# Weight sets split in two pieces at two places of a step, in an attention and two-layer feed-forward kernel with seven-product matrix multiplication

## The chip, the cores and the metric

The kernel runs on one core of a Trainium2 chip. The metric is the device time of one execution in microseconds (us). Three executions of the kernel before took 1682.86, 1685.94 and 1686.4 us; the median is 1685.94.

## The reference

```python
kv = einsum('bhsd,bhse->bhde', k, v)              # batch 8, heads 8, seq 576, head_dim 64
out = einsum('bhsd,bhde->bhse', q, kv)
out = out / sqrt(mean(out * out, -1) + 1e-6) * g_norm
x = out.transpose(0, 2, 1, 3).reshape(4608, 512)
gate = 1 / (1 + exp(-(x @ w_gate)))               # w_gate, w_val: 512 x 1536
y = (gate * (x @ w_val)) @ w_out                  # w_out: 1536 x 512
h = y @ w_in                                      # 512 x 2048
g = where(h >= 1, h, where(h <= -1, 0, (h + 1) ** 2 / 4))
result = g @ w_out2                               # 2048 x 512
```

All of it is float32.

## The kernel before, in words

Each large float32 product is made from three matmuls of rounded parts: an operand is split into a high part (a cast on ScalarE, ACT) and a low part (operand minus high part, on VectorE, DVE), and TensorE (PE) adds low x high, high x low and high x high (`product`). On top of that the four large products are done block by block with seven products of half size instead of eight (numbered 1 to 7, in the order 1, 5, 6, 2, 7, 4, 3), whose operands are sums and differences of quarters. ACT copies some results out of PSUM (`p1_kept`, `u2_kept`, `u3_kept`), DVE adds others (`c11`, `c12`, `c22`).

There are four stages. A: x times w_gate and w_val, 96 steps (16 half blocks of tokens by 6 sets of output columns), with the attention of the next batches between its products in the first seven blocks. B: the gated result times w_out, 8 blocks. C: y times w_in, 64 steps (8 blocks by 8 sets). D: the last product, 18 units.

The sums of weight quarters are made as 34 tasks, one for each *weight set* of seven chunks of 256 columns. GpSimd (POOL) loads a set's four quarters into one of two stage buffers, makes three more chunks out of them in four sums (L657 to L664, L668 to L675), and then loads the set after the next into the buffer that has come free, once `v_ready` says that the set before is done. `split_weights(task)` on ACT (L733) casts the seven chunks of the stage into the ring `v_hi`, in one instruction of 1792 columns (L749); `split_weights(task)` on DVE (L1105) subtracts them into the ring `v_lo`, again in one instruction (L1108, recorded at `low`, L1097), and counts `v_ready` up by one.

The order of each engine is written out by hand; every engine runs its list in order and waits at semaphores. In stage A, ACT's step k is (L892 to L963): copy of product 1 (`p1_kept`, L900), sigmoid of the first half (L903), root or first items of the next block, **the weight set** (L910 to L915), copy of product 6 (`u2_kept`, L924), more items, `square_heads` and `split_square` of attention (L938), sigmoid of the second half (L945, it waits for `c12`), inverse (L947), copy of product 7 (`u3_kept`, L951). DVE's step k is (L1315 to L1405): `c22` (L1321), items, product of the first half (`h0_ready`, L1342), items, **the weight set** (L1357 to L1362), `c12` (L1371), an item, `c11` (L1380), `split_square` (L1382), `split_inverse` (L1384), product of the second half (`h_ready`, L1389), items.

PE's step k in stage A is: (k, 1), (k, 5), (k-1, 4), (k, 6), (k-1, 3), (k, 2), (k, 7), each six matmuls, where (k, n) is product n of step k. (k, 7) waits for `u2_kept`; (k, 5) waits for `c12` of the step before; (k-1, 3) waits for `c22`; attention's products stand between them. In the first six steps of the blocks 0 and 8, (k, 1) waits also for `v_ready`, that is for its own weight set (L1690).

Sets are made at these places: set 0 and set 1 ahead of the loop or in step 0; sets 2 to 5 in the steps 1 to 4 of stage A (the set made in step k is wanted by (k+1, 1)); sets 6 to 11 in the steps 40, 43, 45, 46, 49 and 50 (`SECOND_SETS`, wanted from step 48 on); sets 12 to 25 in fourteen steps from 53 to 87 (`FOLDS`), which SyncE stores to DRAM (L443 to L449) for stages B and D; sets 26 to 29 in stage B; sets 30 to 33 in the steps 0, 1, 3 and 4 of stage C (`THIRD_SETS`, wanted from step 4 on). In stage C the set stands near the end of the step on both engines: on ACT after the copies for `c21` and `u2_kept` (L1043), on DVE after `c12`, the clamp and `c11` (L1512).

Of the kernel before, what the change touches and what calls it, by code (L numbers as in the profile page):

```python
# [27 lines left out]
SEVEN = 7  # L28
# [39 lines left out]
def chunk_pieces(task):  # L68
    if task < A2_TASK:
        return parts(SEVEN * task, SEVEN)  # L70
    if task < FOLD1_TASK:
        return parts(42 + SEVEN * (task - A2_TASK), SEVEN)
    if task < C_TASK:

        return parts(28 + SEVEN * (task % 2), SEVEN)
    return parts(14 + SEVEN * (task - C_TASK), SEVEN)


# [8 lines left out]
def program(nc, kv_in, q_in, qrest_in, g_in, w1_in, w2_in, out):  # L87
# [15 lines left out]
    with ctx:  # L103
# [189 lines left out]
        def heads_of(k):  # L293
# [3 lines left out]
            return (n, c) if 2 <= n < B and c < K else None  # L297

        def mean_of(k):
            return heads_of(k - 1) if k else None  # L300
# [64 lines left out]
        def _(sp):  # L365
# [77 lines left out]
            def store_fold_hi(task):  # L443
                sp.wait_ge(v_hi_done, task + 1)
                sp.dma_start(fold_place(task, 0), fold_chunks(v_hi, task)).then_inc(fold_stored[task % 2], 16)

            def store_fold_lo(task):
                sp.wait_ge(v_ready, task + 1)
                sp.dma_start(fold_place(task, 1), fold_chunks(v_lo, task)).then_inc(fold_stored[task % 2], 16)  # L449
# [114 lines left out]
            for b in range(C_BLOCKS):  # L564

                sp.wait_ge(ct_ready, SEVEN * (b + 1))
                if b < C_BLOCKS - 1:
                    load_block(b + 1)
                else:
                    load_quarter(0, 1)  # L570
                for s in range(C_SETS):

                    if b == C_BLOCKS - 3 and s == 0:
                        sp.wait_ge(v_ready, TASKS)
# [34 lines left out]
        def _(pool):  # L609
# [99 lines left out]
            for task in range(TASKS):  # L709
# [10 lines left out]
                if 0 < task < TASKS - 1:  # L720
                    pool.wait_ge(v_ready, task)
                if task == C_TASK:
# [9 lines left out]
        def _(act):  # L732
            def split_weights(task):  # L733
                act.wait_ge(stage_summed, 4 * (task + 1))
# [11 lines left out]
                elif C_TASK <= task:  # L746
                    act.wait_ge(p_done[ORDER[min(task - C_TASK - 1, 6)]], C0)
                for base, first, count in chunk_pieces(task):
                    done = nc.scalar.copy(v_hi[:, base:base + count, :], stage[:, task % 2, first:first + count, :])  # L749
# [129 lines left out]
            for c in range(1, K):  # L879
                square_heads(0, c)  # L880
            split_weights(0)
            scale_heads(0, 1)
# [5 lines left out]
            for i in range(4):  # L888
                split_item(0, i)
            split_weights(1)  # L890

            for k in range(A_STEPS + 1):  # L892
# [15 lines left out]
                if s == 0 and b < A_BLOCKS:  # L908
                    split_item(b, 4)
                if 1 <= k < 5:  # L910
                    split_weights(1 + k)
                if k in SECOND_SETS:
                    split_weights(A2_TASK + SECOND_SETS[k])
                if k in FOLDS:
                    split_weights(FOLD1_TASK + FOLDS[k])  # L915
                if k == A_STEPS - 1:
# [18 lines left out]
                if k == 1:  # L935
                    square_heads(1, 2)
                    scale_heads(1, 2)
                if heads_of(k):  # L938
                    square_heads(*heads_of(k))
# [27 lines left out]
            for b in range(B_BLOCKS):  # L967
                for i, number in enumerate(ORDER):
# [24 lines left out]
                    if b == B_BLOCKS - 2 and i in (2, 4):  # L993
                        split_weights(C_TASK + i // 2 - 1)
                    if b == B_BLOCKS - 1:
                        if 2 <= i < 4:
                            split_weights(C_TASK + i)
                        elif i == 4:
# [10 lines left out]
            for k in range(C_STEPS + 1):  # L1009
                b, s = divmod(k, C_SETS)  # L1010
                g = C0 + k
                if k < C_STEPS:
                    act.wait_ge(p_done[1], g + 1)
                    act.wait_ge(c11_ready, g)
                    if k == 0:
                        act.wait_ge(c12_ready, C0)
                        act.wait_ge(c22_ready, C0)
                    nc.scalar.copy(c_kept[:, 0, :], X[k % 2][:, 0:C]).then_inc(p1_kept, 1)  # L1018
                if 0 < b < C_BLOCKS and s == 0:
                    split_c_item(b, 4)  # L1020
# [22 lines left out]
                if k in THIRD_SETS:  # L1043
                    split_weights(C_TASK + THIRD_SETS[k])
                if k == 60:
# [49 lines left out]
        def _(dve):  # L1095
# [8 lines left out]

            def split_weights(task):  # L1105
                dve.wait_ge(v_hi_done, task + 1)
                for base, first, count in chunk_pieces(task):
                    done = low(v_lo[:, base:base + count, :], stage[:, task % 2, first:first + count, :],  # L1108
# [185 lines left out]
            copy_kv(0)  # L1294
            split_weights(0)
            invert(0)
# [18 lines left out]
            for k in range(A_STEPS + 1):  # L1315
# [41 lines left out]
                if 1 <= k < 5:  # L1357
                    split_weights(1 + k)
                if k in SECOND_SETS:
                    split_weights(A2_TASK + SECOND_SETS[k])  # L1360
                if k in FOLDS:
                    split_weights(FOLD1_TASK + FOLDS[k])  # L1362
                if k == A_STEPS - 1:
# [21 lines left out]
                if k:  # L1385
                    tile = gate[:, (k - 1) % 2, 1, :]
                    dve.wait_ge(sig1_ready, k)
                    dve.wait_ge(c22_ready, k)
                    nc.vector.tensor_tensor(tile, c22[:], tile, ALU.mult).then_inc(h_ready, 1)  # L1389
                if s == 3 and b + 1 < B:  # L1390
                    normalize(b + 1, 3)
                if k == 0:
                    split_weights(1)
                    sum_item(0, 5)
# [16 lines left out]
            for b in range(B_BLOCKS):  # L1411
                for i, number in enumerate(ORDER):
# [20 lines left out]
                    if b == B_BLOCKS - 2 and i in (2, 4):  # L1433
                        split_weights(C_TASK + i // 2 - 1)
                    if b == B_BLOCKS - 1:
                        if 2 <= i < 4:
                            split_weights(C_TASK + i)
                        elif i == 4:
# [19 lines left out]
            for k in range(C_STEPS + 1):  # L1458
# [28 lines left out]
                elif k == C_STEPS - 2:  # L1487
                    sum_d_item(0, 2)
                if k:
                    dve.wait_ge(p_done[3], g)  # L1490
# [21 lines left out]
                if k in THIRD_SETS:  # L1512
                    split_weights(C_TASK + THIRD_SETS[k])
                if k == C_STEPS - 1:
# [41 lines left out]
        def _(pe):  # L1556
# [125 lines left out]
            def a_product(k, number, dst, start):  # L1682
# [6 lines left out]
                if number == 1 and b in (0, B):  # L1689
                    pe.wait_ge(v_ready, (A_SETS if b else 0) + s + 1)  # L1690
                chunk = ((42 if b >= B else 0) + SEVEN * s) % CHUNKS + QUAD[number]
# [90 lines left out]
            def c_product(k, number, dst, start):  # L1782
# [6 lines left out]
                if number == 1 and b == 0:  # L1789
                    pe.wait_ge(v_ready, C_TASK + s + 1)  # L1790
                chunk = (14 + SEVEN * s) % CHUNKS + QUAD[number]
# [100 lines left out]
```

## Time and profile before

| | |
|---|---|
| the profiled execution's own time | 1682.83 us |
| its span, first to last instruction | 1681.0 us |
| median of three timed executions | 1685.94 us (1682.86 to 1686.4) |
| mean granted PE clock | 0.995 of full |
| busy: ACT, POOL | 886.0 us (53%), 204.1 us (12%) |
| instructions | 31808 |
| DMA | 278.91 MB, 166 GB/s in the mean |

A matmul's duration in the timeline is longer than the distance between two of them, since they are pipelined. What an engine waited for stands in square brackets behind a row, with the us for which it was idle; PEld is PE's weight load, which runs beside the matmuls. L1097, L1100 and L1103 are helpers (a subtraction for a low part, an addition, a difference), so there the tile names say which work it is.

### The profile page before, as it was taken

To read this page: it belongs to the slowest core of one execution; us is meant where nothing else is said; L and a number is where in the kernel's file an instruction comes from. 1 tells how busy PE (TensorE), PEld (TensorE's weight loads), DVE (VectorE), ACT (ScalarE), POOL (GpSimd) and SP (SyncE) were. 2 spreads that over 40 slices of the span, in tenths; PEclk is the share of its full clock that TensorE was granted. 3 is DMA by queue.
4 is the path that set the end of the run, shared out by engine and by line. 5 is a ranking of instruction groups with operands and counts; after the bars stand their busy time and mean duration, and the time that the engine had idled before them with its cause. 6 is when DMAs were issued, how large, how long until landed. Compare 5 with 4: busy or idle time off the path is not lost. (4 is left out here: it accounts for less than half of the span.)

```text
span 1681.0 us, 31808 instructions
## 1 busy us (share of the span) xinstructions
PE 1653.5 (98%) x12473; PEld 1623.5 (97%) x12475; DVE 1219.3 (73%) x1725; ACT 886.0 (53%) x1612; POOL 204.1 (12%) x266
## 2 busy tenths in 40 slices
PE   8999999999999999999999999999999999999999
PEld 6799999999999999999999999999999989999999
DVE  4677776778787675877778887777777677676664
ACT  4666666655555554444445555555555444444442
POOL 3510000015432320200002410000001200000000
PEclk9999999999999999999999999999999999999999
DMA  7544434333776778745443433333438944444450
GB/s 259 161 127 145 149 133 145 116 128 132 249 252 227 246 243 279 245 140 154 130 141 139 163 128 131 117 121 141 165 141 272 334 151 138 140 135 126 126 131 34
DMA packets 229317, 278.91 MB, mean 166 GB/s; under 512 B 33072, under 2 KB 172848, under 8 KB 229168
## 3 DMA queue, kind: packets, MB, share of 16 engines
q1 hardware_dynamic: 217104, 233.35, 42.1%
q0 software_dynamic: 12064, 43.52, 7.9%
q8 instruction: 99, 1.62, 0.4%
q14 instruction: 50, 0.41, 0.1%
HBM read 156.76 MB, written 120.06 MB: 165 GB/s over the span
## 5 line engine op out<-in xcount | busy, mean ns | idle before, releaser
L1560 PE MATMUL x<-t_hi,v_lo 128*128 128x288 f32 x1664 | 497.0, 299 | 4.9 <-ACT c_kept L1018 1.8
L1561 PE MATMUL x<-t_lo,v_hi 128*128 128x288 f32 x1664 | 491.9, 296 | 0.0
L1562 PE MATMUL x<-t_hi,v_hi 128*128 128x288 f32 x1664 | 490.4, 295 | 0.0
L1560 PEld LDWEIGHTS x<-t_hi,v_lo 128*128 128x128 f32 x1664 | 313.0, 188 | 9.6 <-issue 2.6
L1562 PEld LDWEIGHTS x<-t_hi,v_hi 128*128 128x128 f32 x1664 | 314.2, 189 | 0.0
L1561 PEld LDWEIGHTS x<-t_lo,v_hi 128*128 128x128 f32 x1664 | 313.6, 188 | 0.1
L1560 PE MATMUL y<-t_hi,v_lo 128*128 128x288 f32 x832 | 248.8, 299 | 5.0 <-DVE c L1100 1.7
L1561 PE MATMUL y<-t_lo,v_hi 128*128 128x288 f32 x832 | 245.9, 295 | 0.0
L1562 PE MATMUL y<-t_hi,v_hi 128*128 128x288 f32 x832 | 245.2, 295 | 0.0
L1560 PE MATMUL x<-v_hi,t_lo 128*128 128x256 f32 x576 | 164.2, 285 | 4.2 <-ACT o_tile L1089 4.2
L1560 PEld LDWEIGHTS y<-t_hi,v_lo 128*128 128x128 f32 x832 | 156.4, 188 | 9.5 <-DVE c_tile L1100 3.1
L1561 PE MATMUL x<-v_lo,t_hi 128*128 128x256 f32 x576 | 163.9, 285 | 0.0
L1562 PE MATMUL x<-v_hi,t_hi 128*128 128x256 f32 x576 | 163.9, 285 | 0.0
L1562 PEld LDWEIGHTS y<-t_hi,v_hi 128*128 128x128 f32 x832 | 156.9, 189 | 0.0
L1561 PEld LDWEIGHTS y<-t_lo,v_hi 128*128 128x128 f32 x832 | 156.6, 188 | 0.1
L1097 DVE TENSOR_TENSOR t_lo<-gq,t_hi 128x1024 fp32r<-128x1024 f32 x90 | 109.7, 1222 | 61.3 <-ACT t_hi L872 61.3
L1097 DVE TENSOR_TENSOR t_lo<-hq,t_hi 128x864 fp32r<-128x864 f32 x112 | 118.3, 1080 | 30.3 <-ACT t_hi L841 30.3
L841 ACT CAST t_hi<-hq 128x864 fp32r<-128x864 f32 x112 | 99.8, 917 | 50.6 <-DVE hq L1103 25.7
L1560 PEld LDWEIGHTS x<-v_hi,t_lo 128*128 128x128 f32 x576 | 111.6, 194 | 4.4 <-ACT o_tile L1089 4.4
L1561 PEld LDWEIGHTS x<-v_lo,t_hi 128*128 128x128 f32 x576 | 111.6, 194 | 0.0
L1562 PEld LDWEIGHTS x<-v_hi,t_hi 128*128 128x128 f32 x576 | 111.5, 194 | 0.0
L872 ACT CAST t_hi<-gq 128x1024 fp32r<-128x1024 f32 x90 | 94.5, 1050 | 31.5 <-PE y L1562 23.4
(185 smaller groups left out, 3518.8 us busy)
## 6 DMA issues: line engine op xcount, KB each, us to landing
g_scratch<-c_tile SPq DMA_DIRECT2D x128, 288.0 KB, 2.4
gq<-g_scratch SPq DMA_DIRECT2D x64, 512.0 KB, 6.1
h_scratch<-gate SPq DMA_DIRECT2D x192, 144.0 KB, 1.9
hq<-h_scratch SPq DMA_DIRECT2D x32, 864.0 KB, 5.2
stage<-w_in POOLq DMA_DIRECT2D x68, 256.0 KB, 3.8
kv_ring<-kv_in SPq DMA_DIRECT2D x30, 512.0 KB, 4.4
fold_hi<-v_hi SPq DMA_DIRECT2D x14, 896.0 KB, 5.0
fold_lo<-v_lo SPq DMA_DIRECT2D x14, 896.0 KB, 6.7
```

Of the source, the lines that this page charges most:

```text
L841: nc.scalar.copy(b_slot(e)[0], b_source(i, hh)).then_inc(bt_hi_done, 1)
L872: nc.scalar.copy(d_slot(e)[0], d_source(u, i)).then_inc(s_hi_done, 1)
L1097: return nc.vector.tensor_tensor(out, raw, hi.bitcast(f32), ALU.subtract)
L1560: nc.tensor.matmul(dst, s_lo, m_hi, start=start, stop=False, skip_group_check=True)
L1561: nc.tensor.matmul(dst, s_hi, m_lo, start=False, stop=False, skip_group_check=True)
L1562: return nc.tensor.matmul(dst, s_hi, m_hi, start=False, stop=stop, skip_group_check=True)
```

## The change

`set_pieces(task, piece)` cuts the chunks of a set at the fourth: piece 0 is four chunks (1024 columns), piece 1 three chunks (768 columns). `split_weights` on both engines takes a piece and handles it alone. `v_hi_done` and `v_ready` now count pieces, so all that wait for a set wait for twice the number; DVE's piece waits for ACT's same piece. In stage A piece 0 stands where the set stood, and piece 1 later in the step: on ACT after the items and attention's extra work of step 1, ahead of `square_heads`; on DVE after the product of the second half (L1389) and ahead of `normalize(b + 1, 3)` and the last items. In stage C piece 1 stands where the set stood, and piece 0 earlier: on ACT right after the copy of product 1 (L1018), on DVE ahead of `c12`. Sets 0, 1 and 26 to 29 are made in two pieces at their one place.

```diff
+def set_pieces(task, piece):
+    low, high = ((0, 4), (4, SEVEN))[piece]
+    cut = [(base, first, max(first, low), min(first + count, high)) for base, first, count in chunk_pieces(task)]
+    return [(base + start - first, start, end - start) for base, first, start, end in cut if end > start]
...
+        def weight_task(k):
+            if 1 <= k < 5:
+                return 1 + k
+            if k in SECOND_SETS:
+                return A2_TASK + SECOND_SETS[k]
+            return FOLD1_TASK + FOLDS[k] if k in FOLDS else None
...
             def store_fold_hi(task):
-                sp.wait_ge(v_hi_done, task + 1)
+                sp.wait_ge(v_hi_done, 2 * (task + 1))
             def store_fold_lo(task):
-                sp.wait_ge(v_ready, task + 1)
+                sp.wait_ge(v_ready, 2 * (task + 1))
...
                 if 0 < task < TASKS - 1:
-                    pool.wait_ge(v_ready, task)
+                    pool.wait_ge(v_ready, 2 * task)
...
-            def split_weights(task):
+            def split_weights(task, piece):
...
-                for base, first, count in chunk_pieces(task):
+                for base, first, count in set_pieces(task, piece):
                     done = nc.scalar.copy(v_hi[:, base:base + count, :], stage[:, task % 2, first:first + count, :])
                 done.then_inc(v_hi_done, 1)
...
# ACT, stage A: in place of the set
+                if weight_task(k) is not None:
+                    split_weights(weight_task(k), 0)
...
                 if k == 1:
                     square_heads(1, 2)
                     scale_heads(1, 2)
+                if weight_task(k) is not None:
+                    split_weights(weight_task(k), 1)
                 if heads_of(k):
                     square_heads(*heads_of(k))
...
# ACT, stage C
                     nc.scalar.copy(c_kept[:, 0, :], X[k % 2][:, 0:C]).then_inc(p1_kept, 1)
+                if k in THIRD_SETS:
+                    split_weights(C_TASK + THIRD_SETS[k], 0)
...
                 if k in THIRD_SETS:
-                    split_weights(C_TASK + THIRD_SETS[k])
+                    split_weights(C_TASK + THIRD_SETS[k], 1)
...
# DVE
-            def split_weights(task):
-                dve.wait_ge(v_hi_done, task + 1)
-                for base, first, count in chunk_pieces(task):
+            def split_weights(task, piece):
+                dve.wait_ge(v_hi_done, 2 * task + piece + 1)
+                for base, first, count in set_pieces(task, piece):
...
# DVE, stage A: piece 0 in place of the set, and
                     nc.vector.tensor_tensor(tile, c22[:], tile, ALU.mult).then_inc(h_ready, 1)
+                if weight_task(k) is not None:
+                    split_weights(weight_task(k), 1)
                 if s == 3 and b + 1 < B:
                     normalize(b + 1, 3)
...
# DVE, stage C
                 elif k == C_STEPS - 2:
                     sum_d_item(0, 2)
+                if k in THIRD_SETS:
+                    split_weights(C_TASK + THIRD_SETS[k], 0)
                 if k:
                     dve.wait_ge(p_done[3], g)
...
                 if k in THIRD_SETS:
-                    split_weights(C_TASK + THIRD_SETS[k])
+                    split_weights(C_TASK + THIRD_SETS[k], 1)
...
# PE, stages A and C
-                    pe.wait_ge(v_ready, (A_SETS if b else 0) + s + 1)
+                    pe.wait_ge(v_ready, 2 * ((A_SETS if b else 0) + s + 1))
-                    pe.wait_ge(v_ready, C_TASK + s + 1)
+                    pe.wait_ge(v_ready, 2 * (C_TASK + s + 1))
```

## Rows read from the trace of the kernel before

**Rows 1.** The page, busy time of the engines: us, share of the span, instructions.

```profile
PE 1653.5 (98%) x12473; PEld 1623.5 (97%) x12475; DVE 1219.3 (73%) x1725; ACT 886.0 (53%) x1612; POOL 204.1 (12%) x266
```

**Rows 2.** Busy us (instructions) of PE, PEld, DVE, ACT, POOL in a window; PEclk; DMA; GB/s.

```profile
1000.00:1070.00 70.00, 70.00 (x527) 70.00 (x526) 52.23 (x79) 38.05 (x71) 0.00 (x0) 1.00 0.39 144
```

**Rows 3.** Waits of PE over the span: releaser, us in all, times, longest.

```profile
PE y L1560 <- DVE c L1100: 1.7, 2, 1.6
...
PE x L1560 <- DVE v_lo L1097: 1.3, 2, 0.7
...
PE y L1560 <- DVE gate L1100: 1.3, 2, 1.1
```

**Rows 4.** Groups by line and shape: count, busy us, mean ns, idle us before.

```profile
L1097 DVE TENSOR_TENSOR t_lo<-gq,t_hi 128x1024 fp32r<-128x1024 f32 x90 | 109.7, 1222 | 61.3 <-ACT t_hi L872 61.3
...
L872 ACT CAST t_hi<-gq 128x1024 fp32r<-128x1024 f32 x90 | 94.5, 1050 | 31.5 <-PE y L1562 23.4 <-DVE gq L1103 6.3 <-PE h L1562 1.8
...
L1097 DVE TENSOR_TENSOR v_lo<-stage,v_hi 128x1792 fp32r<-128x1792 f32 x34 | 70.3, 2068 | 14.7 <-ACT v_hi L749 14.7
...
L749 ACT CAST v_hi<-stage 128x1792 fp32r<-128x1792 f32 x34 | 57.3, 1686 | 2.0 <-POOL stage L664 1.9
...
L1100 DVE TENSOR_TENSOR gate<-y,kept 128x288 f32<-128x288 f32 x96 | 43.2, 450 | 53.3 <-PE y L1562 53.3
```

**Rows 5.** Timeline, end of step 2 of stage A: start us, us, instruction, idle before.

```profile
62.89 1.95 DVE L1097 TENSOR_TENSOR v_lo<-stage,v_hi 128x1792 fp32r<-128x1792 f32 x1
...
65.24 0.45 ACT L945 ACTIVATE gate<-gate 128x288 f32<-128x288 f32 x1 [1.25 <-DVE gate L1100]
...
65.43 0.29 PE L1560 MATMUL x<-t_hi,v_lo 128*128 128x288 f32 x1
...
66.52 0.46 DVE L1389 TENSOR_TENSOR gate<-c,gate 128x288 f32<-128x288 f32 x1
...
66.55 0.53 PE L1648 MATMUL h<-inv_pair,spread_r 48*128 48x288 f32 x2 [0.16 <-DVE inv_pair L1097]
```

**Rows 6.** Timeline, step 4 of stage A.

```profile
81.07 2.57 DVE L1097 TENSOR_TENSOR v_lo<-stage,v_hi 128x1792 fp32r<-128x1792 f32 x1
...
81.71 2.51 POOL L660 TENSOR_TENSOR stage<-stage 128x256 f32<-128x256 f32 x1
...
82.36 0.67 ACT L780 CAST ps_hi<-sq 128x576 fp32r<-128x576 f32 x1
...
83.78 0.37 PE L1560 MATMUL x<-t_hi,v_lo 128*128 128x288 f32 x1 [0.71 <-DVE v_lo L1097]
...
84.29 1.25 DVE L1097 TENSOR_TENSOR ps_lo<-sq,ps_hi 128x576 fp32r<-128x576 f32 x1
...
85.59 0.34 PE L1633 MATMUL m<-ps_lo,head_r 128*48 128x288 f32 x1 [0.78 <-DVE ps_lo L1097]
```

**Rows 7.** Timeline, steps 59 and 60 of stage A.

```profile
466.98 0.40 PE L1560 MATMUL y<-t_hi,v_lo 128*128 128x288 f32 x1 [1.09 <-DVE gate L1100]
...
467.81 0.75 DVE L1097 TENSOR_TENSOR t_lo<-t_sum,t_hi 128x576 fp32r<-128x576 f32 x1
...
468.70 0.37 PE L1560 MATMUL x<-t_hi,v_lo 128*128 128x288 f32 x1
```

**Rows 8.** Timeline, steps 1, 4 and 5 of stage C.

```profile
952.22 0.37 PE L1560 MATMUL y<-t_hi,v_lo 128*128 128x288 f32 x1 [1.52 <-DVE t_lo L1097]
...
970.96 0.30 PE L1560 MATMUL x<-t_hi,v_lo 128*128 128x288 f32 x1
...
971.28 1.69 ACT L749 CAST v_hi<-stage 128x1792 fp32r<-128x1792 f32 x1 [1.61 <-POOL stage L664]
...
975.39 0.40 PE L1560 MATMUL x<-t_hi,v_lo 128*128 128x288 f32 x1 [0.56 <-ACT c_kept L1018]
```

**Rows 9.** Windows behind two long waits, columns as in rows 2.

```profile
668.00:675.00 7.00, 4.81 (x23) 4.45 (x23) 5.74 (x10) 3.09 (x6) 1.51 (x3) 0.76 0.36 110
...
947.00:953.00 6.00, 3.24 (x23) 2.80 (x22) 3.42 (x4) 2.69 (x4) 1.09 (x2) 1.00 0.07 15
```

More of the change, by code:

```diff
@@ L573, in _ @@
                     if b == C_BLOCKS - 3 and s == 0:
-                        sp.wait_ge(v_ready, TASKS)
+                        sp.wait_ge(v_ready, 2 * TASKS)
                         all_stored(sp, g_stored, C_SETS * b, 32)
@@ L880, in _ @@
                 square_heads(0, c)
-            split_weights(0)
+            split_weights(0, 0)
+            split_weights(0, 1)
             scale_heads(0, 1)
@@ L889, in _ @@
                 split_item(0, i)
-            split_weights(1)
+            split_weights(1, 0)
+            split_weights(1, 1)
             for k in range(A_STEPS + 1):
@@ L909, in _ @@
                     split_item(b, 4)
[L910 to L915, printed above, removed]
+                if weight_task(k) is not None:
+                    split_weights(weight_task(k), 0)
                 if k == A_STEPS - 1:
@@ L993, in _ @@
                     if b == B_BLOCKS - 2 and i in (2, 4):
-                        split_weights(C_TASK + i // 2 - 1)
+                        for piece in range(2):
+                            split_weights(C_TASK + i // 2 - 1, piece)
                     if b == B_BLOCKS - 1:
                         if 2 <= i < 4:
-                            split_weights(C_TASK + i)
+                            for piece in range(2):
+                                split_weights(C_TASK + i, piece)
                         elif i == 4:
@@ L1294, in _ @@
             copy_kv(0)
-            split_weights(0)
+            split_weights(0, 0)
+            split_weights(0, 1)
             invert(0)
@@ L1356, in _ @@
                         sum_item(b + 1, 5)
[L1357 to L1362, printed above, removed]
+                if weight_task(k) is not None:
+                    split_weights(weight_task(k), 0)
                 if k == A_STEPS - 1:
@@ L1389, in _ @@
                     nc.vector.tensor_tensor(tile, c22[:], tile, ALU.mult).then_inc(h_ready, 1)
+                if weight_task(k) is not None:
+                    split_weights(weight_task(k), 1)
                 if s == 3 and b + 1 < B:
@@ L1392, in _ @@
                 if k == 0:
-                    split_weights(1)
+                    split_weights(1, 0)
+                    split_weights(1, 1)
                     sum_item(0, 5)
@@ L1433, in _ @@
                     if b == B_BLOCKS - 2 and i in (2, 4):
-                        split_weights(C_TASK + i // 2 - 1)
+                        for piece in range(2):
+                            split_weights(C_TASK + i // 2 - 1, piece)
                     if b == B_BLOCKS - 1:
                         if 2 <= i < 4:
-                            split_weights(C_TASK + i)
+                            for piece in range(2):
+                                split_weights(C_TASK + i, piece)
                         elif i == 4:
```

## The prediction

> **What bounds the kernel now.** Read the page's first part first: TensorE (PE) is busy for 98% of the span [rows 1], so of 1681.0 us it stands still for 27.5. The other engines matter only where PE waits for them. Where it does not wait, a matmul costs 70.00/527 = 0.133 us [rows 2] and a product of six 0.80. Next, the waits of PE, a short list: for a weight set's low part, which is what this change moves, twice, 1.3 us together; for a gate half, 1.3 us; for `c22` twice, 1.7 us, of which 1.6 is one wait near the end of stage A [rows 3]. What a better place for the pieces could win is in such lines. Last, the order of time around the steps that hold a weight set: what PE is given next, and how early it was ready. I call product n of step k (k, n).
>
> **The operations.** A whole set is 1792 columns, one cast of 1686 ns on ScalarE and one subtraction on VectorE, 2068 ns in the mean. The first piece is 1024 columns; the trace has this shape as a cast of 1050 ns and a subtraction of 1222 ns; an addition such as `c12` takes 450 ns [rows 4]. The 768 columns between the two shapes cost 0.83 ns each on ScalarE and 1.10 on VectorE; so the second piece, 256 columns fewer than the first, is 1050-212 = 840 ns and 1222-282 = 940 ns. The sums are 1.89 against 1.69 us and 2.16 against 2.07: 34 sets make +6.8 and +3.1 us of busy time. Neither engine sets the end (53% and 73% of the span [rows 1]), so this costs only where one of them is late. No set wraps round the ring of 56 chunks (all bases are multiples of 7), so each piece is one instruction. The doubled counts ask for the whole set as before: PE, SyncE's stores and GpSimd's next load all wait for the second piece.
>
> What counts is the place. In VectorE's order the first piece stays ahead of the additions that PE waits for (`c12`, `c11`), which can come 0.8 us earlier; the second piece moves behind them and behind the product of the second half (L1389), which waits for ScalarE's second sigmoid. GpSimd gets the stage buffer 1 to 3 us later, and has the room: a set is loaded two sets ahead.
>
> **Step 2 of stage A.** The set made here is wanted by the first product of step 3. Before, the subtraction starts at 62.89 and ends at 64.84, and (3,1) starts at 65.43 without a wait [rows 5]. After: first piece until 64.1, `c12` until 64.5, `c11` until 64.9; the sigmoid starts at 64.6 instead of 65.24; from its start to that of L1389 there were 1.28 us (the inverse's cast and subtraction lie between), so L1389 starts at 65.9 and ends at 66.3, the second piece at 67.2. (3,1) starts at 67.3, 1.9 later. Behind it PE waited 0.3 us for the inverse (65.43+0.80 = 66.23, started 66.55), which is then ready: net **+1.6**. It is at least 1.2, if additions and inverse gain 0.4 more than I gave them, and at most 2.2, if L1389 gets no earlier at all: 66.52+0.46+0.94 = 67.9.
>
> **Step 4.** Here PE already waits 0.71 us for the low part and starts (5,1) at 83.78; then it waits 0.78 for the low part of the squares, until 85.59 [rows 6]. After: first piece 81.07 to 82.3, both additions until 83.1. On ScalarE the second cast stands ahead of the squares; the first ends 0.64 earlier, the second adds 0.84, so their high part ends at 83.2 where it ended at 83.03. Their subtraction (0.75 if undisturbed) ends at 84.1, L1389 at 84.6, the second piece at 85.4 to 85.5. (5,1) starts there, 1.6 to 1.7 later, but the mean square can follow 0.80 behind it, at 86.2 instead of 85.59: **+0.6**. Bounds: +0.3, if these operations overlap more than their durations say; +1.3, if a GpSimd sum comes between.
>
> On that there is a row and a rule. GpSimd's 256-column sum at 81.71 took 2.51 us, and the subtraction beside it 2.57, where the mean is 2.07 [rows 4, 6]: they hold each other up. The Trainium skill, page "SBUF — State Buffer", section "SBUF: two separate sides", says that VectorE instructions with two SBUF inputs and GpSimd's share one port pair as an exclusive lock, kept for a whole instruction. By that rule, the trace agreeing with it, cutting the subtraction gives GpSimd a gap to get in, and the second piece could wait for one more sum; this step would be nearer its upper bound.
>
> **Steps 0, 1 and 3.** Step 0 makes its set in two pieces in one place, and PE waits for it: +0.1 (0 to 0.2). By the reckoning of step 2 the second piece ends in step 1 just when (2,1) can start (0 to +0.4), and in step 3 well before (4,1), which has attention's products ahead of it: 0 for both. For set 0 the root leads on, not the set: 0.
>
> **Later sets of stage A.** All are made at least three steps ahead of use, so the late second piece harms nothing directly. What could be won is a wait of PE behind a long subtraction. The largest, 1.09 us at 466.98 (step 59), is for `c12`, queued behind it [rows 7]. With the first piece alone `c12` comes 0.8 earlier and PE starts (60,5) at 466.2. But two products later (60,6) started at 468.70, right after VectorE's next item (467.81+0.75 = 468.56), and VectorE has the same work before that item, plus 0.1 us. So the wait only moves: 0, between -0.2 and +0.2; likewise in step 53. In step 46 the shorter of the two `c22` waits (1.7-1.6 = 0.1 [rows 3], and as much again for the restart) goes, since the set no longer pushes what follows: -0.3, at least 0.
>
> **The start of stage C.** Set 30's subtraction began after a wait for a store; `c22` and an item stood behind it, and PE waited 1.52 us until 952.22 [rows 8]. The first piece now lies in the time in which VectorE waits anyway, so (0,3) starts about 1.1 earlier (the second piece alone, 0.94, stands before `c22`, instead of 2.07), and GpSimd loads as much earlier. But set 33, in step 4 of this stage, waits 1.61 us for GpSimd's last sum, until 971.28; its cast stood behind the copies for `c21` and `u2_kept`, and now its first piece stands ahead of them. With the sum 1.1 earlier the piece ends at 971.2, the copies at 972.0, and (4,7), which started at 970.96, starts there. Then (5,1), (5,5), (4,4) follow without gaps, and (5,6) starts at 972.0+3.2 = 975.2 against 975.39, where the 0.56 before it goes. Of the 1.1, 0.2 is left, and GpSimd's sums may fall better: **-0.3**, bounds -1.1 (sum 0.9 earlier still) and +0.7 (sum hardly earlier).
>
> **Sum.** 1.6+0.6+0.1-0.3-0.3 = +1.7 us. The profiled execution took 1682.83 us (span 1681.0), so 1684.5 in its state; it lies at the lowest of the three timed runs, 3.1 below their median of 1685.94. On the median it is 1687.6. All lower bounds give -0.1, all upper ones +5.0. The sum is within 0.2% (3.4 us), about what a measurement of this kernel can tell from no change.
>
> **Rivals.**
> - *The clock falls.* Behind the wait of 1.6 us near 670 [rows 3] the granted clock averaged 0.76 over 7 us, so 1.7 us of full speed were lost in a stretch at 1.2 instead of 2.4 GHz; behind the 1.52 us at 952 it did not fall [rows 9]. The new wait in step 2, or that in step 4, can do the same: +1.7+1.7 = +3.4, with both +5.1. This is the case on the slower side, and it decides from one fall on. The Trainium skill, page "TensorE: Matmul & The Clock Gate", section on the clock gate, calls the low level the default, which activity releases; both rows are open to that, and it names no other price here. The 3.1 us between timed runs may be such falls.
> - *Slower by the waits alone.* Steps 2 and 4 and stage C at their upper bounds, 2.2+1.3+0.7, and nothing won in step 46: +4.3. For it: GpSimd's held-up sum [rows 6, 8]. Against: three bounds at once.
> - *Faster.* The waits at 467 and 952 go and nothing comes behind them (-0.8, -1.5), that of 0.56 at 975 too, with -0.3 of step 46, and steps 0, 2 and 4 cost their lower bounds, +1.5: -1.7; with one clock fall of the span missing (1.7), -3.4, just where it would be told as faster. Against: the item behind 467 [rows 7], the sum at 971 [rows 8].
> - *Nothing:* the second pieces of steps 2 and 4 are hidden after all, 0. Against: (3,1) started 0.6 us after the low part, and the second piece moves behind three operations [rows 5].
>
> **Chances.** Forecast (+1.7, from -0.1 to +3.3) 0.60; clock fall 0.17, of it 0.09 beyond 3.4; slower by the waits alone 0.08; faster 0.07, of it 0.04 at 3.4 or beyond; nothing 0.08. So faster 0.04, slower 0.17, same 0.79. Range 1683.5 to 1690.8: from 1 below the forecast in the profiled execution's state to the median with the higher clock case nearly in full.
>
> **What would show it.** Right: a wait of PE for `v_lo` of some 1.5 to 2 us near 65 to 67 and another near 84; the wait at 467 short, with one for `t_lo` two products on; the wait at 952 below 0.6 us, and one near 970 for the copy of L1033; 68 casts and 68 subtractions of about 1.05/0.84 and 1.22/0.94. Wrong: (3,1) without a wait; no wait at 970; the wait at 467 gone with none behind it.

## The result and the profile after

The changed kernel took 1690.49 us (median of 11 runs, 1684.48 to 1692.97), the kernel before 1683.63 us (median of 11, 1678.05 to 1689.45). The ratio is 1.0033, 95% interval 1.0020 to 1.0046: slower by 0.33%, some 5.6 us. The forecast was +1.7 us and "within 0.2%"; the time lies inside the range given (1683.5 to 1690.8), 0.3 us below its upper end.

The profile is of an execution of 1684.48 us, the shortest of the eleven. Its mean granted clock was 0.997; in the others it was 0.991 (1692.97 us) to 0.996, which is 1.4 us for each 0.001; a line through all runs, each kernel about its own mean, has the same slope. The two profiled executions differ by 1.65 us where the medians differ by 6.9. In the trace before the granted clock was at its lower level for 3.4 us from 29.5, 36.3 and 671.2 us and for 6.8 us from 1350.4; in the trace after for 3.4 us from 44.5, 88.9 and 1355.3. So the trace after is one with few such falls: it shows the places where time went, not how often the clock falls.

The page, busy time of the engines:

```profile
PE 1651.2 (98%) x12473; PEld 1621.3 (96%) x12475; DVE 1221.7 (73%) x1759; ACT 891.5 (53%) x1646; POOL 203.4 (12%) x266
```

Waits of PE over the span (releaser, us in all, times, longest). The two waits for `v_lo` of 1.3 us together [rows 3] have become three of 6.4:

```profile
PE x L1584 <- DVE v_lo L1117: 6.4, 3, 3.5
...
PE x L1584 <- DVE t_lo L1117: 2.2, 3, 1.6
PE m L1604 <- DMA kv_ring<-kv_in: 2.2, 1, 2.2
...
PE y L1584 <- DVE c L1120: 1.9, 2, 1.6
...
PE x L1584 <- ACT c_kept L1053: 1.2, 1, 1.2
```

Groups by shape (count, busy us, mean ns, idle us before). The casts add 6.6 us to ScalarE (35.5+28.4-57.3), as forecast. The subtractions add 11.0 to VectorE (42.3+39.0-70.3), where 3.1 were forecast: the second piece takes 1146 ns in the mean, not 940 (worked out from [rows 4]). Of the 34 second pieces 21 took 0.95 us and one 1.13; twelve took 1.47 to 1.49, and each of these began 0.15 to 0.3 us after a sum of GpSimd had begun. VectorE's busy time as a whole rose by 2.4 us only, since other instructions were held up less (L1389, now L1406: 48.5 us before, 45.5 after, for 96):

```profile
L1117 DVE TENSOR_TENSOR v_lo<-stage,v_hi 128x1024 fp32r<-128x1024 f32 x34 | 42.3, 1243 | 8.4 <-ACT v_hi L765 8.4
L1117 DVE TENSOR_TENSOR v_lo<-stage,v_hi 128x768 fp32r<-128x768 f32 x34 | 39.0, 1146 | 0.0
...
L765 ACT CAST v_hi<-stage 128x1024 fp32r<-128x1024 f32 x34 | 35.5, 1044 | 2.3 <-POOL stage L679 2.3
...
L765 ACT CAST v_hi<-stage 128x768 fp32r<-128x768 f32 x34 | 28.4, 836 | 0.0
```

**Step 2 of stage A.** VectorE and, last, PE on the timeline (start us, us, instruction, idle before). This answers to [rows 5]: both additions, the inverse, the second product (L1406), and only then the second piece, for which (3,1) waits:

```profile
63.64 1.15 DVE L1117 TENSOR_TENSOR v_lo<-stage,v_hi 128x1024 fp32r<-128x1024 f32 x1
64.71 0.44 DVE L1120 TENSOR_TENSOR gate<-y,kept 128x288 f32<-128x288 f32 x1
...
65.98 0.52 DVE L1117 TENSOR_TENSOR inv_pair<-inv,inv_pair 16x288 fp32r<-16x288 f32 x1 [0.47 <-ACT inv_pair L821]
66.54 0.46 DVE L1406 TENSOR_TENSOR gate<-c,gate 128x288 f32<-128x288 f32 x1
66.91 0.95 DVE L1117 TENSOR_TENSOR v_lo<-stage,v_hi 128x768 fp32r<-128x768 f32 x1
...
68.01 0.37 PE L1584 MATMUL x<-t_hi,v_lo 128*128 128x288 f32 x1 [1.68 <-DVE v_lo L1117]
```

**Step 4.** The same, with GpSimd's sums beside it; it answers to [rows 6]. Three VectorE operations that overlap a sum are long (1.01, 0.97, 1.47 us), and (5,1) waits 3.55 us. The last row is of the trace before, where L1389 was as long beside a sum:

```profile
83.49 1.22 DVE L1117 TENSOR_TENSOR v_lo<-stage,v_hi 128x1024 fp32r<-128x1024 f32 x1
...
85.59 1.01 DVE L1117 TENSOR_TENSOR ps_lo<-sq,ps_hi 128x576 fp32r<-128x576 f32 x1 [0.15 <-ACT ps_hi L796]
86.53 0.97 DVE L1406 TENSOR_TENSOR gate<-c,gate 128x288 f32<-128x288 f32 x1
87.43 1.47 DVE L1117 TENSOR_TENSOR v_lo<-stage,v_hi 128x768 fp32r<-128x768 f32 x1
...
85.46 0.99 DVE L1389 TENSOR_TENSOR gate<-c,gate 128x288 f32<-128x288 f32 x1
```

```profile
85.95 1.24 POOL L677 TENSOR_TENSOR stage<-stage 128x256 f32<-128x256 f32 x1
87.27 0.82 POOL L679 TENSOR_TENSOR stage<-stage 128x256 f32<-128x256 f32 x1
```

```profile
89.05 0.58 PE L1584 MATMUL x<-t_hi,v_lo 128*128 128x288 f32 x1 [3.55 <-DVE v_lo L1117]
89.42 0.44 PE L1585 MATMUL x<-t_lo,v_hi 128*128 128x288 f32 x1
```

The matmul at 89.42 takes 0.44 us where others take 0.29: the clock has fallen, from 88.9 on, just before the wait ended. The window around it (columns as in [rows 2]) has a mean granted clock of 0.57; over 9 us around the end of step 2's wait it stayed whole:

```profile
66.00:75.00 9.00, 7.32 (x48) 6.12 (x47) 5.91 (x12) 3.25 (x7) 3.41 (x6) 1.00 0.54 178
...
88.50:92.50 4.00, 3.45 (x15) 3.31 (x16) 2.77 (x5) 0.74 (x2) 1.09 (x2) 0.57 0.78 214
```

What step 4 cost in all shows between two products of attention that lie ahead of it and behind it. In the trace before (the first two rows) they start at 79.72 and 103.76, 24.04 us apart; here (the other two) 26.04 apart, so **+2.0**:

```profile
79.72 0.29 PE L1560 MATMUL h<-pq_hi,kv_lo 128*128 128x288 f32 x1
...
103.76 0.29 PE L1560 MATMUL h<-pq_hi,kv_lo 128*128 128x288 f32 x1
...
82.14 0.29 PE L1584 MATMUL h<-pq_hi,kv_lo 128*128 128x288 f32 x1
...
108.18 0.29 PE L1584 MATMUL h<-pq_hi,kv_lo 128*128 128x288 f32 x1
```

**Stage C.** The products that answer to [rows 8], and the cast of set 33. The first row is of the trace before:

```profile
949.64 0.40 PE L1560 MATMUL x<-t_hi,v_lo 128*128 128x288 f32 x1 [1.24 <-ACT c_kept L1018]
...
953.07 0.40 PE L1584 MATMUL x<-t_hi,v_lo 128*128 128x288 f32 x1
...
954.57 0.37 PE L1584 MATMUL y<-t_hi,v_lo 128*128 128x288 f32 x1 [0.44 <-DVE t_lo L1117]
...
974.36 0.40 PE L1584 MATMUL x<-t_hi,v_lo 128*128 128x288 f32 x1 [1.17 <-ACT c_kept L1053]
...
977.90 0.40 PE L1584 MATMUL x<-t_hi,v_lo 128*128 128x288 f32 x1
```

```profile
972.66 1.05 ACT L765 CAST v_hi<-stage 128x1024 fp32r<-128x1024 f32 x1 [2.28 <-POOL stage L679]
```

From the product ahead of (0,3) to (5,6) it is 977.90-953.07 = 24.83 us; before, that product started at 949.64, so 975.39-949.64 = 25.75. Stage C gained 0.9 there, and 0.3 more in two short stops of PE before the products behind that are gone: **-1.2**. The wait for a copy near 974 is there, as forecast. The 1.24 us that PE waited just ahead of the product at 949.64 are gone too, but the change has no part in that: of the fourteen traces of this case six have this wait (1.1 to 1.7 us), e4 below among them, which is the change but for two guards, and eight don't, e11 among them, whose stage C is that of before.

**A wait that nobody expected.** In the trace after, VectorE waited 2.26 us near 647 for a store of a gate tile to land, and the products behind it came 1.0 us later:

```profile
647.20 0.46 DVE L1120 TENSOR_TENSOR gate<-z,kept 128x288 f32<-128x288 f32 x1 [2.26 <-DMA h_scratch<-gate]
```

It costs 0.8 to 1.4 us in six of the fourteen traces (the change, e3, e4, e5, e7, e9) and is in none of the others. e5 has all sets of stage A whole, so the late pieces don't make it; what these six share is the set of step 4 of stage C in two places, 300 us later. Why the store lands late stays open.

### The profile page after: what moved, and what is told of

It is laid out like the page before. It is cut to its first block and busy times, and to the rows that moved or that the text cites. A ratio compares the mean times of both kernels' runs of the same rounds, so it can differ in the third digit from the quotient of the medians.

```text
span 1682.7 us, 31904 instructions
## 1 busy us (share of the span) xinstructions
PE 1651.2 (98%) x12473; PEld 1621.3 (96%) x12475; DVE 1221.7 (73%) x1759; ACT 891.5 (53%) x1646; POOL 203.4 (12%) x266
```

## The experiments

Each kernel is the change with up to four settings: APART_A, the steps of stage A whose set has its second piece at the late place (in the others the pieces stand one behind the other at the early place, on ScalarE and VectorE); APART_C, the same for steps 0, 1, 3, 4 of stage C; WHOLE, the sets that stay one instruction and count for two; and the guards of GpSimd's sums of sets 1 and 2 (`pool.wait_ge(v_ready, 1)` and `2`). The change had left these two counts as they were, so set 2's sums began when half as much was done: at 32.91 us in the trace after, at 42.10 in that of before. A run's ratio is to the kernel before on the same chip. The medians of before were 1683.17, 1687.56 and 1684.28 us for the first, second and third group of four.

| kernel | median us | ratio, 95% | wait for `v_lo`, step 2 | step 4 | start of a clock fall at step 4's wait |
|---|---|---|---|---|---|
| the change | 1690.49 | 1.0033 (1.0020..1.0046) | 1.68 | 3.55 | 88.9 us |
| e1_together | 1686.09 | 1.0020 (1.0009..1.0031) | none | 1.32 | none |
| e2_early | 1689.21 | 1.0028 (1.0015..1.0041) | 1.68 | 3.55 | 89.1 |
| e3_no_early | 1683.04 | 0.9999 (0.9988..1.0010) | none | 1.31 | none |
| e4_guard | 1689.11 | 1.0030 (1.0017..1.0043) | 1.61 | 3.55 | 89.9 |
| e5_c_only | 1685.17 | 0.9992 (0.9978..1.0006) | none | 0.70 | none |
| e6_whole01 | 1684.07 | 0.9991 (0.9979..1.0002) | none | 1.31 | none |
| e7_pool | 1691.04 | 1.0037 (1.0021..1.0052) | 1.67 | 2.23 | 87.0 |
| e8_step4 | 1686.70 | 1.0005 (0.9990..1.0020) | none | 3.58 | 87.5 (6.8 us long) |
| e9_after_c11 | 1685.40 | 1.0005 (0.9992..1.0018) | 0.20 | 1.46 | none |
| e10_best | 1682.30 | 0.9985 (0.9972..0.9998) | none | 0.70 | none |
| e11_step2 | 1683.70 | 1.0002 (0.9986..1.0018) | 1.61 | 0.70 | none |
| e12_together2 | 1686.48 | 1.0010 (0.9996..1.0024) | none | 1.31 | none |

**First group: which of the places costs.**

```
e1_together:  APART_A = ()                 APART_C = ()            guards 2 and 4
```

> Every set in two pieces, but both pieces at the one place where the whole set stood, and GpSimd's two guards ahead of sets 1 and 2 doubled like all other counts. So only the instruction count differs from the kernel before. Theory A (the late second pieces of steps 2 and 4 of stage A cost the time): within 1 us of the kernel before, ratio 0.9995 to 1.0008. Theory B (68 more instructions and the cuts themselves cost): most of the measured 5.6 us, ratio about 1.003. Theory C (GpSimd's guards, which the change left at 1 and 2): as A, 1.000.

```
e2_early:     APART_A = (1, 2, 3, 4)       APART_C = ()            guards 2 and 4
```

> As the kernel with both pieces together, but in the steps 1 to 4 of stage A the second piece stands late, as in the change. Theory A: this alone brings the whole loss, ratio 1.002 to 1.0045; its trace has a wait of the tensor engine for v_lo of 1.5 to 2 us near 66 and one of 2.5 to 3.7 near 85. Theory B: ratio as of both pieces together, plus nothing. Theory C: 1.000 to 1.001.

```
e3_no_early:  APART_A = all but 1 to 4     APART_C = (0, 1, 3, 4)  guards as in the change
```

> The change, but in the steps 1 to 4 of stage A both pieces stand together in the old place. Theory A: the loss is gone and the gain of stage C is left, ratio 0.998 to 1.000; no wait for v_lo above 1 us near 66 and 85. Theory B: still 1.003. Theory C (guards, as in the change): still about 1.003.

```
e4_guard: the change, and in GpSimd's loop
-                    pool.wait_ge(v_ready, 1)
+                    pool.wait_ge(v_ready, 2)
...
-                    pool.wait_ge(v_ready, 2)
+                    pool.wait_ge(v_ready, 4)
```

> The change, but GpSimd's two guards wait for 2 and 4 pieces, that is for the whole sets 0 and 1 as before. Theory A: as the change, ratio 1.002 to 1.0045, with the waits for v_lo near 66 and 85. Theory C (the sums of set 2, which ran at 33 to 37 us instead of 42 to 46 and slowed three subtractions from 0.75 to 1.28 us, cost the time): 1.000 to 1.001.

Without the late pieces of steps 1 to 4 the whole loss is gone (e3, 0.9999, its interval clear of that of the change and of e4); with them and no other late piece it is nearly all there (e2, 1.0028). The guards are worth nothing that shows (e4 as the change). e1, with no piece at a late place, is still 0.2% slower, so the medians of e1 and e2 alone would leave little for the late pieces. Its trace is 3.5 us longer than that of before, and 2.6 of that arise in the first 62 us, where it waits 3.6 us for `kv_ring` against 0.8. These first 62 us differ from those of before by -1.2 (e3) to +7.3 us (e9) among the traces, whatever the pieces do. e1 was run again below.

**Second group: stage C, the first sets, and what is in step 4.**

```
e5_c_only:    APART_A = ()    APART_C = (0, 1, 3, 4)   WHOLE = sets 0 to 29           guards 2 and 4
```

> Only stage C's sets 30 to 33 in two pieces at two places; all others whole as in the kernel before. Theory A (early sets cost, stage C gains, the rest is neutral): ratio 0.998 to 1.000, and stage C's first six steps 1 to 2.5 us shorter; set 33's first piece waits for GpSimd and the tensor engine waits 1.2 us for the copy of product 6 near 970. My prediction had -0.3 us for stage C. Theory D (cutting set 0 lets GpSimd load set 2 earlier, against attention's kv loads): does not apply here, no kv wait above 1 us near 34.

```
e6_whole01:   APART_A = ()    APART_C = ()             WHOLE = sets 0 and 1           guards 2 and 4
```

> Both pieces together in one place everywhere, but sets 0 and 1 whole as before. The kernel with all pieces together measured 1.0020, with a wait of 3.6 us for kv_ring near 36. Theory D (the cut of set 0 ends it 0.5 us earlier, GpSimd's load of set 2 starts earlier and kv_ring's loads land later): ratio 0.9995 to 1.0005 here, kv wait back to 0.8 us. Theory B (more instructions cost): 1.002 as with all together. Theory E (the kv wait varies from run to run whatever the sets do): 1.002, with any kv wait.

```
e7_pool: the change, and GpSimd's sums of set 6 wait until set 5 is done
                 elif task == 2:
                     pool.wait_ge(v_ready, 2)
+                elif task == A2_TASK:
+                    pool.wait_ge(v_ready, 2 * A2_TASK)
```

> The change, but GpSimd makes the sums of set 6 only after set 5 is wholly done, so none of its sums runs beside step 4's second piece. Theory A1 (the order of VectorE's list costs, GpSimd's sums lengthen it by 1 us, and a fall of the clock follows the wait of 3.7 us): the wait for v_lo near 85 goes from 3.7 to 2.3 to 2.9 us; the fall of the clock near 89 stays or goes; ratio 1.001 to 1.003. Theory A2 (GpSimd is no part of it): wait 3.7 and ratio as the change, 1.003.

```
e8_step4:     APART_A = (4,)  APART_C = ()             WHOLE = all sets but set 5     guards 2 and 4
```

> All sets whole as in the kernel before but set 5, whose second piece stands late in step 4. Theory A: the wait for v_lo near 83 to 87 is 3 to 3.7 us with a fall of the clock behind it, +2 us or ratio 1.001 to 1.002. If the wait of step 2 is needed for the size of that of step 4: wait about 2.5, ratio 1.000 to 1.001.

e7 separates what made step 4's wait so long. Its VectorE and PE rows, with no sum beside them:

```profile
85.06 0.76 DVE L1132 TENSOR_TENSOR ps_lo<-sq,ps_hi 128x576 fp32r<-128x576 f32 x1
85.73 0.45 DVE L1425 TENSOR_TENSOR gate<-c,gate 128x288 f32<-128x288 f32 x1
86.10 0.95 DVE L1132 TENSOR_TENSOR v_lo<-stage,v_hi 128x768 fp32r<-128x768 f32 x1
```

```profile
87.20 0.58 PE L1605 MATMUL x<-t_hi,v_lo 128*128 128x288 f32 x1 [2.23 <-DVE v_lo L1132]
```

0.76, 0.45 and 0.95 us against 1.01, 0.97 and 1.47 of the changed kernel, 1.29 us together; the wait is shorter by 1.32. So the sums made 1.3 us of it. But the time didn't come back (its ratio, 1.0037, is even above the 1.001 to 1.003 expected): the clock fell all the same,

```profile
86.80:90.20 3.40, 3.00 (x12) 2.86 (x13) 3.33 (x5) 0.95 (x3) 3.00 (x3) 0.53 0.56 178
```

and a wait of 1.28 us for `pq_lo` near 101 us came in. The two attention products are 26.33 us apart (81.61, 107.94), no less than in the changed kernel. The sums had only moved: they now ran beside the subtraction for `pq_lo`, which took 1.27 us instead of 0.75. What such a hold-up costs the kernel, other traces show: in the five where `pq_lo` was held up without a late piece in step 4 (e3, e5, e6, e11, e12; waits of 1.28 to 1.30 us) the two products are 24.33 to 24.46 us apart, in the four where it was not (before, e1, e9, e10; 0.58) 23.98 to 24.05. So it costs 0.3 to 0.4 us. e8 has the fall with set 5's late piece alone:

```profile
88.97 0.58 PE L1603 MATMUL x<-t_hi,v_lo 128*128 128x288 f32 x1 [3.58 <-DVE v_lo L1130]
```

```profile
87.20:94.00 6.80, 5.03 (x21) 4.88 (x22) 4.00 (x6) 1.19 (x3) 2.51 (x5) 0.52 0.47 157
```

its distance is 26.99 us. Its ratio (1.0005) can't be told from that of no change, so for step 4 alone the trace is the evidence, not the median.

e5 (0.9992) came out as expected, with the waits of stage C as in the change. e6 (0.9991) came out just below the 0.9995 to 1.0005 expected, but not for the reason given: its wait for `kv_ring` was 1.8 us, not back to 0.8.

**Third group: order or place, the best version, and the repeat.**

```
e9_after_c11: the change, and in VectorE's loop of stage A
+                if 1 <= k < 5:
+                    split_weights(weight_task(k), 1)
                 if heads_of(k):
                     split_square(*heads_of(k))
...
-                if weight_task(k) is not None:
+                if weight_task(k) is not None and k >= 5:
                     split_weights(weight_task(k), 1)
```

> The change, but in steps 1 to 4 of the run-in VectorE makes the second piece of the subtraction right after the item's combining addition (c11), ahead of the split of the squares (split_square), split_inverse and the second product. Theory 'order' (the loss of steps 2 and 4 comes from where the second piece stands behind VectorE's other work of the item): the wait for v_lo near 66 us falls from 1.68 to 0.3 to 0.8 us, that near 85 us from 3.55 to 1.2 to 1.6 us, there is no stretch at half the clock near 89 us, and the ratio to before is 0.9985 to 1.001. Rival (the two places cost by themselves, by contention or by the cast, wherever VectorE's piece stands): a wait of over 2.5 us near 85 to 89 us and the clock fall stay, and the ratio is 1.003 as that of the change.

```
e10_best:     APART_A = ()    APART_C = (0, 1, 3)      WHOLE = sets 0 to 29 and 33    guards 2 and 4
```

> All sets whole at their old place as before, but sets 30, 31 and 32 of the start of stage C made at two places, and set 33 whole at its old place (GpSimd's guards doubled, so its sums run where they did before). Theory (the change's only gain is the start of stage C, about 1.2 us from step C0 to C8, and set 33's own late first piece costs part of it): that stretch at 45.0 to 46.2 us against 47.36 before, no wait for v_lo near 970 us, and a ratio of 0.998 to 0.9995. Rival (what stage C gains is lost again in a later wait): 1.000.

```
e11_step2:    APART_A = (2,)  APART_C = ()             WHOLE = all sets but set 3     guards 2 and 4
```

> All sets whole as before, but set 3 alone with its second piece late in step 2 of the run-in. Theory (step 2 costs by itself what the changed profile shows, a wait for v_lo of 1.68 us at 68 us, and no clock fall follows a wait of this length): a wait of 1.6 to 1.7 us near 66 to 68 us, the stretch from step 2 to step 4 about 1.1 us longer than 18.8 us, no clock fall between 66 and 75 us, and a ratio of 1.0003 to 1.001. Rival (the wait only takes the place of others): the stretch the same within 0.3 us and a ratio of 1.000.

```
e12_together2: as e1_together
```

> The same kernel as e1_together, run again: every set's cast and subtraction cut into four and three chunks, the two pieces one right after the other at the old place. It came out at 1.0020 [1.0009, 1.0031] the first time. If cutting itself costs that, it is 1.0015 to 1.0025 again; if that was the spread of the start of the kernel (waits for the first transfers and the clock falls of the first 50 us), it is 0.999 to 1.001.

In e9 the second piece stands right behind the addition for `c11`, and PE's two waits shrink to 0.20 (less than the 0.3 to 0.8 expected) and 1.46 us:

```profile
73.06 0.37 PE L1605 MATMUL x<-t_hi,v_lo 128*128 128x288 f32 x1 [0.20 <-DVE v_lo L1130]
```

```profile
90.40 1.45 DVE L1130 TENSOR_TENSOR v_lo<-stage,v_hi 128x768 fp32r<-128x768 f32 x1
91.78 1.28 DVE L1130 TENSOR_TENSOR ps_lo<-sq,ps_hi 128x576 fp32r<-128x576 f32 x1
```

```profile
92.00 0.37 PE L1605 MATMUL x<-t_hi,v_lo 128*128 128x288 f32 x1 [1.46 <-DVE v_lo L1130]
```

```profile
88.00:96.00 8.00, 6.45 (x48) 5.99 (x47) 8.00 (x11) 5.30 (x12) 5.63 (x6) 1.00 0.69 241
```

The clock stayed whole and the attention products are 23.98 us apart (87.19, 111.17), as before the change. The second piece is as long as ever here (1.45 us, a sum beside it), and ScalarE's casts stand where the change put them: what mattered was what VectorE had ahead of the piece. The ratio (1.0005) is lower than that of the change, with intervals that just don't touch. e11 has step 2 alone: a wait of 1.61 us, +1.6 us over the step where 1.1 was expected, no fall, nothing that the median can show. e10 beats the kernel before by 0.15%, with an interval that ends at 0.9998, close to no change. From the product ahead of (0,3) to (5,6) it takes 976.36-952.66 = 23.70 us, 2.05 less than before:

```profile
952.66 0.40 PE L1603 MATMUL x<-t_hi,v_lo 128*128 128x288 f32 x1 [1.70 <-ACT c_kept L1047]
...
976.36 0.40 PE L1603 MATMUL x<-t_hi,v_lo 128*128 128x288 f32 x1 [0.38 <-ACT c_kept L1047]
```

With set 33 whole at its old place the copy that (4,7) wants stands ahead of the cast, and the wait of 1.17 us is gone. Counted from ahead of the wait that precedes the first product (1.70 us here, 1.24 before), it is 1.6 us less. e8 and e11, whose stage C is that of before, differ from it by 0.2 and 0.5 us over the same stretch. The repeat of e1 came out at 1.0010 where 1.0020 stood, between the two outcomes that I had set apart: it doesn't settle whether cutting alone costs.

## Why the prediction was right, and where it was wrong

The direction and the places were right, and the measured time is inside the range with luck. The case held most likely (+1.7, up to +3.3, at 0.60) is not what came: by the ratio the time moved by 5.6 us, beyond even the case with two clock falls (+5.1, all clock cases together at 0.17), of which the trace shows one. The range reached far enough because its upper end was that case on top of 1685.94, the median of the first three runs of the kernel before, where all eleven have 1683.63.

- **Step 2, +1.6.** Right in kind and size. L1406 and the second piece came as reckoned (2.90 us from the start of the first piece to that of L1406, forecast 3.0; 0.46 and 0.95 us), (3,1) was 1.8 us late, where 1.9 was forecast, and some 0.2 us were won back where the wait for the inverse went: +1.7 over the whole step, and +1.6 in e11, with this late piece alone.
- **Step 4, +0.6.** The step that failed: it took VectorE's operations at their undisturbed times, and it put the fall of the clock at nothing in the sum. (5,1) was forecast 1.6 to 1.7 later and came 2.8 later. Undisturbed it would have been 1.5 (e7: a wait of 2.23 against 0.71 [rows 6]); GpSimd's sums added 1.3. The trace before had the sign of that in the same step, 1.25 us for the subtraction of the squares [rows 6] and 0.99 for L1389. The later waits were absorbed by this one, those for `ps_lo` and `pq_lo` (0.78 and 0.58 before), so the waits alone make some +0.5: of the 2.0 us, the time lost at the low clock, twelve distances of 0.24 us between matmuls instead of 0.13 and 0.2 at the first, is 1.5. This is an account of one trace; no kernel here has a wait of 2.2 us or more in step 4 without a fall. The size of the term for the waits was right by two errors that met, a delay 1.2 us longer than forecast and more waits behind it that took it up. The rival that stood beside it with 0.17, the fall of the clock, is what happened here, in all five kernels with the piece at the late place in step 4.
- **The rule on the shared port.** The prediction gave it as an upper bound of +1.3 through one more sum between the pieces. The hold-up came (1.3 us, e7), and its price could not be told apart from the fall in step 4; where `pq_lo` alone was held up, it was 0.3 to 0.4 us. The Trainium skill, page "SBUF — State Buffer", section "SBUF: two separate sides", says that of a VectorE instruction with two SBUF inputs and one of GpSimd the one that starts first keeps the shared ports for its whole length. The trace agrees: the second piece took 1.47 us, having begun 0.16 us after a sum, and 0.95 without one, and the twelve long pieces all began behind a sum. The same holds for L1406, which reads two SBUF tiles of 288 columns: 0.97 beside a sum against 0.45.
- **Steps 0, 1, 3, +0.1.** No wait for `v_lo` at the end of steps 1 and 3. The wait for the set of step 0, near 41 us, was 1.19 us against 0.57, but e10, with this set whole, has 0.94; the start of the kernel differs by more than the term between executions (a wait for `kv_ring` of 0.8 us before and 2.2 after, falls at other places).
- **Steps 59 and 46.** In step 59 the wait moved, as forecast: `c12` came in time, and the next product but one waited for its item, which stood behind the second piece. It costs 0.5 more than the wait that it replaced (1.56 against 1.09), where 0.2 was the bound: the piece took 1.49 us instead of 0.94. The wait that it replaced is itself not steady: 0.3 to 1.7 us in the kernels that keep these sets in one place. Step 46 gave nothing; a wait of 0.3 us for `c22` stayed (1.9 us in two, one of 1.6).

```profile
471.47 1.49 DVE L1117 TENSOR_TENSOR v_lo<-stage,v_hi 128x768 fp32r<-128x768 f32 x1
472.88 0.75 DVE L1117 TENSOR_TENSOR t_lo<-t_sum,t_hi 128x576 fp32r<-128x576 f32 x1
```

```profile
473.78 0.37 PE L1584 MATMUL x<-t_hi,v_lo 128*128 128x288 f32 x1 [1.56 <-DVE t_lo L1117]
```

- **Stage C, -0.3.** The mechanism was right (the wait at 952 shrank from 1.52 to 0.44, one near 974 for the copy came in) and the size too small: -1.2, just beyond the lower bound. The 0.9 of it up to (5,6) stands in e3, e4 and e9 as well. From the product ahead of (0,3), GpSimd's last sum for set 33 ended 971.28-949.64 = 21.6 us later before and 972.66-953.07 = 19.6 later after, 2.0 us earlier, where I had given it 1.1. e3 and e5 have the same waits in stage C (0.44 and 1.18; 0.33 and 1.18).
- **"The doubled counts ask for the whole set as before".** Wrong for GpSimd: two of its guards were not doubled. e4 shows that it had no price.
- **The sum.** Both kernels run the same matmuls in the same order, so the start of one and the same matmul can be compared along the two traces. The difference after minus before grows and shrinks like this:

| stretch | us |
|---|---|
| the start, up to 62 us | +0.7 |
| step 2 | +1.7 |
| step 4, its fall of the clock included | +2.0 |
| step 59 | +0.5 |
| the wait for a store near 647 | +1.0 |
| no fall of the clock behind the wait for `c22` near 675 | -1.4 |
| no wait for a copy ahead of the product at 949.64 | -1.3 |
| the start of stage C | -1.2 |
| all the rest | -0.3 |

The four places that the prediction named make +3.0 us against the +1.7 forecast; the others make -1.3 in this pair of traces, and they vary among the fourteen traces for other reasons than the late pieces. That both sum up to +1.7 us, the forecast, is luck. The medians differ by more, and the clock is a part of it. The mean granted clock over all runs was 0.9939 in the changed kernel, 0.9948 in e4 and 0.9940 in e2, against 0.9963 in e3, the same kernel without the late pieces of steps 1 to 4. At 1.4 us for each 0.001 that is an estimated 2.1 us (e4, measured beside e3) to 3.4 us (the change) of the 5.2 and 5.7 us between the ratios. The traces of e2, e4 and e7, with the same late pieces, have 17 to 20.5 us at the low clock against 10.2 in that of the change: more of it between 31.8 and 41.4 us in all three, near 956 in e2 and e7, and twice as long near 1357 in e4 and e7. How often each of these falls comes, one trace of a kernel can't tell. That, and the 0.1 to 0.2% of e1 and e12, stays open. e6, with sets 0 and 1 whole and the others cut, was at 0.9991, which points to the start of the kernel: its interval is clear of that of e1 but overlaps that of e12.

## What to carry to other kernels

When an instruction is cut so that its second half yields to others, list what stands ahead of the half in its engine's order and who waits for the set as a whole; where the consumer is the next step, put the half behind only the one operation that is urgent (here the addition for `c11`), not at the end of the step. Where a change makes TensorE wait longer, price a fall of its clock on top as a case of its own (here 1.5 us in step 4, in all five kernels where that wait reached 2.2 us). A cut pays only where the whole instruction held something up (three sets of stage C here), so do it for those alone. Where counts of a semaphore change, look for every wait on it, those with a constant too.

## What the runs showed of the hardware

- *Falls of the clock.* At step 4's wait the granted clock fell to the 1.2 GHz level in all five kernels where the wait was 2.23 to 3.58 us, and in none of the nine where it was 0.70 to 1.46. At step 2's wait of 1.61 to 1.68 us it fell in none of five. The same wait of 1.6 us for `c22` near 675 us stands in all fourteen traces; a fall went with it in before, e1, e6 and e10 and none in the other ten. One of 1.8 us near 45 stands in all fourteen as well, with a fall in six. And a wait of 2.2 us for `kv_ring` near 35 brought none in the change nor in e12. So the length of a wait alone doesn't decide it. The fall of 3.4 us in step 4 cost 1.5 us.
- *A fall can begin inside a wait.* In e8 it began at 87.5, 1.5 us ahead of the matmul that ended the wait of 3.58 us, and lasted 6.8 us. In the change, e4 and e7 the fall began 0.1 to 0.3 us before the wait in step 4 ended, in e2 as it ended.
- *VectorE instructions that begin behind a sum of GpSimd are held up, long or short.* 288 columns took 0.97 us instead of 0.45, 576 columns 1.01 instead of 0.76, 768 columns 1.47 instead of 0.95: each lost 0.25 to 0.5 us, so a short one loses the larger share. Cutting an instruction moved these hold-ups more than it added to them: the second pieces lost some 6.7 us to them in all, but VectorE's busy time rose from 1219.3 to 1221.7 us only.
